# Three stacked half terms per head for the score products of batches 2 to 4

## The reference

```
for t in range(S):
    m_new = maximum(f[t] + m, i[t]); f_stab = exp(f[t] + m - m_new); i_stab = exp(i[t] - m_new)
    C = f_stab * C + i_stab * outer(v[t], k[t]);  n = f_stab * n + i_stab * k[t]
    y[t] = sigmoid(o[t]) * (C @ q[t]) / maximum(abs(n . q[t]), 1)
h = relu(x^T @ w_tok1) @ w_tok2;  u = x + h^T;  out = u + relu(u @ w_ch1) @ w_ch2
```

## Time and profile before

| | |
|---|---|
| median of three runs | 459.25 us (458.14 to 460.07) |
| the profiled execution, its own time | 460.83 us |
| its span, first to last instruction | 459.1 us |
| mean granted TensorE clock | 0.996 |
| PE busy | 440.7 us, 96% |
| DVE / ACT / POOL busy | 259.1 / 209.4 / 209.1 us |
| DMA | 47.38 MB, 103 GB/s on average |
| chain that ended last | PE 83%, issue 6%, DVE 4%, ACT 3%, POOL 2% |

### The profile page before, as it was taken

The page is one execution under the profiler, slowest core; times in us unless marked ns, Lnnn a source line. Parts: engine busy times, 40 slices in busy tenths (PEclk is TensorE's granted clock), DMA queues, the critical chain, the costliest instruction groups (busy, mean ns, idle before and its releaser), DMA issues.

```text
span 459.1 us, 9511 instructions
## 1 busy us (share of the span) xinstructions
PE 440.7 (96%) x3463; PEld 407.9 (89%) x3463; DVE 259.1 (56%) x592; ACT 209.4 (46%) x517; POOL 209.1 (46%) x293
## 2 busy tenths in 40 slices
PE   7899989998999998999999998999999998999996
PEld 3587878998999997999999997899999997999996
DVE  8588965678865346776663236677674326222212
ACT  3665449665555247655552136755552213211120
POOL 7524410888886242988871204698883000000000
PEclk9899999999999999999999999999999999999999
DMA  7666991343344414544344013444410010000101
GB/s 215 191 172 192 348 256 39 104 115 129 95 134 136 140 44 115 148 127 131 127 152 141 1 44 87 144 135 140 126 60 1 1 43 1 0 2 0 45 1 43
DMA packets 36617, 47.38 MB, mean 103 GB/s; under 512 B 3357, under 2 KB 29083, under 8 KB 36571
## 3 DMA queue, kind: packets, MB, share of 16 engines
q1 hardware_dynamic: 35674, 45.76, 33.1%
q10 hardware_dynamic: 896, 1.02, 0.6%
HBM read 42.73 MB, written 4.03 MB: 102 GB/s over the span
## 4 chain that ended last, share of the span: by engine, by line
PE 83%; issue 6%; DVE 4%; ACT 3%; POOL 2%; DMA 1%; ACTq 0%; DVEq 0%; POOLq 0%
PE pC L1151 32%; PE pA L1222 7%; PE pA L1223 7%; PE pA L1224 7%; PE pS L1063 6%; PE pA L1151 5%; PE pY L1120 4%; PE pA L1226 3%; PE pA L1227 3%; PE pY L1099 2%; PE pN L1075 2%; DMA x<-o_gate_dram 1%; PE pA L1181 1%; POOL vw L517 1%; DVE pb L860 1%
## 5 line engine op out<-in xcount | busy, mean ns | idle before, releaser
L974 DVE SCALAR_TENSOR_TENSOR h_lo<-pA,h_hi 128x384 fp32r<-128x384 f32 x96 | 53.5, 557 | 148.0 <-ACT h_hi L755 147.9
L755 ACT ACTIVATE h_hi<-pA 128x384 fp32r<-128x384 f32 x96 | 46.9, 489 | 138.7 <-PE pA L1227 138.6
L1151 PE MATMUL pC<-wc_hi,h_hi 128*128 128x320 f32 x288 | 94.1, 327 | 0.8 <-DVE wc_lo L841 0.8
L1151 PE MATMUL pC<-wc_lo,h_hi 128*128 128x320 f32 x288 | 88.7, 308 | 0.0
L1151 PE MATMUL pC<-wc_hi,h_lo 128*128 128x320 f32 x288 | 88.5, 307 | 0.0
L489 POOL TENSOR_TENSOR gb<-gb,pb 128x384 f32<-128x384 f32 (+1 forms) x54 | 51.7, 957 | 65.7 <-ACT pb L623 65.4
L1222 PE MATMUL pA<-uT_hi,wc_hi 128*128 128x384 f32 x192 | 65.3, 340 | 1.9 <-DVE uT_hi L952 1.9
L1223 PE MATMUL pA<-uT_lo,wc_hi 128*128 128x384 f32 x192 | 64.7, 337 | 0.0
L1224 PE MATMUL pA<-uT_hi,wc_lo 128*128 128x384 f32 x192 | 64.3, 335 | 0.0
L1151 PEld LDWEIGHTS pC<-wc_hi,h_hi 128*128 128x128 f32 x288 | 54.0, 188 | 2.1 <-DVE h_lo L974 1.1
L1151 PEld LDWEIGHTS pC<-wc_lo,h_hi 128*128 128x128 f32 x288 | 54.2, 188 | 0.1
(11 more groups left out here) (128 smaller groups left out, 885.0 us busy)
## 6 DMA issues: line engine op xcount, KB each, us to landing
gb<-g_dram SPq DMA_DIRECT2D x18, 512.0 KB, 4.0
kv<-kvN_dram SPq DMA_DIRECT2D x24, 324.0 KB, 4.1
kd<-kT_dram SPq DMA_DIRECT2D x24, 180.0 KB
qz<-qT_dram SPq DMA_DIRECT2D x72, 60.0 KB
out_dram<-u SPq DMA_DIRECT2D x24, 160.0 KB, 1.9
qd<-qT_dram SPq DMA_DIRECT2D x20, 180.0 KB, 2.6
gq<-g_dram SPq DMA_DIRECT2D x45, 60.0 KB
wc_raw<-w_ch_dram SPq DMA_DIRECT2D x6, 384.0 KB, 5.8
```

The lines of the kernel that those rows point to most:

```text
L755: nc.scalar.activation(h2[0][:, slot % 2], pA[slot % 2][:, 0:HALF], ACT.Relu).then_inc(h2_hi, 1)
L974: nc.vector.scalar_tensor_tensor(h2[1][:, slot % 2], pA[slot % 2][:, 0:HALF], 0.0, h2[0][:, slot % 2].bitcast(F32), ALU.max, ALU.subtract) ...
L1151: ins = mm(dst, a[p], b[q], start=first and n == 0, stop=last and n == 2)
```

## The change

Batch 0 keeps the plain product. For batches 1 to 3 the host lays keys and queries out a second time (array kq): per head 120 rows, which hold the 40 components three times over, the middle copy split around row 64, as `order` says. On the chip the whole 120 rows are rounded to fp32r (kq_stack), then rows 0 to 39 of the keys and rows 64 to 103 of the queries are overwritten with their low halves (raw minus rounded). One fp32r product over 120 rows then sums key-low x query-high, high x high and key-high x query-low. It is one product of 128 x 128 per head, three (or two) per step, in place of one float32 product of 384 (or 256) columns.

```diff
+FIRST_PREPARED = 3
+PREPARES_AT = 2
+TWO_AT = 6
+K_LOW, Q_LOW = slice(0, D), slice(64, 64 + D)
...
-        gq = sb("gq", [ROWS, Q, NG, L])
+        gq = sb("gq", [ROWS, R, NG, L])
+        kq_raw = sb("kq_raw", [ROWS, NG, 2, GH, L])
+        kq_stack = sb("kq_stack", [ROWS, NG, 2, GH, L], F32R)
...
+        def prepares(ba, m):
+            if m < PREPARES_AT:
+                return []
+            steps = [m + 1] if m < TWO_AT else [m + 1, m + 2] if m == TWO_AT else [m + 2]
+            n = STEPS + (FIRST_PREPARED if ba < B - 1 else 0)
+            return [later(ba, k) for k in steps if k < n and later(ba, k) >= FIRST_PREPARED]
...
+            def load_step(ba, m):                      # SP
+                c, g = divmod(m, NG)
+                k = later(ba, m)
+                if k < NG:
+                    sp.wait_ge(s_mm, STEPS)
+                elif k < NG + FIRST_PREPARED:
+                    sp.wait_ge(kq_first, 2 * (k - NG + 1))
+                else:
+                    sp.wait_ge(kq_lo, k - NG - FIRST_PREPARED + 1)
+                    sp.wait_ge(kq_low_keys, k - NG - FIRST_PREPARED + 1)
+                sp.dma_start(kq_raw[:, g], kq[ba - 1, c, :, g]).then_inc(kq_in[g], 16)
...
+            def load_two_steps(ba, c):
+                load_step(ba, NG * c)
+                load_step(ba, NG * c + 1)
             def load_rest(ba, c):
-                if ba > 0:
-                    load_decays(ba, c)
                 load_values(ba, c)
+                load_decays(ba, c)
+                load_step(ba, NG * c + 2)
                 if c > 0:
-                    load_inter(ba, c)
+                    load_query_decays(ba, c)
+                    load_queries(ba, c)
             def load_chunk(ba, c):
-                load_scores(ba, c)
+                load_two_steps(ba, c)
                 load_rest(ba, c)
...
             def rest(ba, m):                           # POOL
+                sixteen_bits(ba, m)                    # the old body of rest
+                for k in prepares(ba, m):
+                    low_keys(k)
+            def low_keys(k):
+                raw, stack = step_tiles(kq_raw, k % NG), step_tiles(kq_stack, k % NG)
+                pool.wait_ge(kq_hi, k - FIRST_PREPARED + 1)
+                nc.gpsimd.tensor_tensor(stack[0][K_LOW], raw[0][K_LOW], stack[0][K_LOW].bitcast(F32),
+                                        ALU.subtract).then_inc(kq_low_keys, 1)
...
+                    if n == NC:                        # ahead of batch 1's first rest
+                        for m in range(FIRST_PREPARED):
+                            prepare_first(m)           # copy 120x768 and both low halves, all on POOL
...
+                for k in prepares(ba, m):              # ACT, in attention(ba, m), after chunk_start and v_middle
+                    step_high(k)
+            def step_high(k):
+                g = k % NG
+                act.wait_ge(kq_in[g], 16 * (k // NG + 1))
+                act.wait_ge(s_mm, STEPS + k - NG + 1)
+                nc.scalar.activation(kq_stack[:, g, :, 0:HEADS[g], :], kq_raw[:, g, :, 0:HEADS[g], :],
+                                     ACT.Copy).then_inc(kq_hi, 1)
...
+                    for k in prepares(ba, m):          # DVE, in attention(ba, m), after p_low(m-1)
+                        step_low(k)
+            def step_low(k):
+                raw, stack = step_tiles(kq_raw, k % NG), step_tiles(kq_stack, k % NG)
+                dve.wait_ge(kq_hi, k - FIRST_PREPARED + 1)
+                nc.vector.tensor_tensor(stack[1][Q_LOW], raw[1][Q_LOW], stack[1][Q_LOW].bitcast(F32),
+                                        ALU.subtract).then_inc(kq_lo, 1)
...
+            def step_scores(ba, m):                    # PE, from batch 1 on
+                g = m % NG
+                k = later(ba, m)
+                if k < FIRST_PREPARED:
+                    pe.wait_ge(kq_first, 2 * (k + 1))
+                else:
+                    pe.wait_ge(kq_lo, k - FIRST_PREPARED + 1)
+                    pe.wait_ge(kq_low_keys, k - FIRST_PREPARED + 1)
+                pe.wait_ge(p_ready, STEPS + k)
+                for j in range(HEADS[g]):
+                    last = mm(scores_bank(ba, m)[:, j * L:(j + 1) * L], kq_stack[:, g, 0, j, :], kq_stack[:, g, 1, j, :],
+                              start=True, stop=True)
+                last.then_inc(s_mm, 1)
...
+        order = np.r_[0:D, 0:64 - D, 0:D, 64 - D:D]    # host
```

More of the change, by code:

```diff
@@ L163, in program, with gq_at, step_tiles @@
         pN = bank("pN")
+        def gq_at(ba, c):
+            if ba == 0:
+                return gq_first[:, :, :] if c % Q == R else gq[:, c % Q]
+            return gq[:, c % R]
+        def step_tiles(tensor, g):
+            return [tensor[:, g, side, 0:HEADS[g], :] for side in range(2)]
         def scores_bank(ba, m):
@@ L179, in program @@
         gb_in = [sem(f"gb_in{i}") for i in range(Q)]
-        gq_in = [sem(f"gq_in{i}") for i in range(Q)]
+        gq_in = [sem(f"gq_in{i}") for i in range(R)]
+        kq_in = [sem(f"kq_in{i}") for i in range(NG)]
+        kq_hi = sem("kq_hi")
+        kq_lo = sem("kq_lo")
+        kq_low_keys = sem("kq_low_keys")
+        kq_first_hi = sem("kq_first_hi")
+        kq_first = sem("kq_first")
         g_out = sem("g_out")
@@ L416, in _ @@
                 if b < B - 2:
-                    load_scores(b + 2, 0)
+                    load_two_steps(b + 2, 0)
                 store(b, 0)
@@ L562, in attention @@
                         x_low(ba, c - 1)
+                for k in prepares(ba, STEPS):
+                    low_keys(k)
                 x_low(ba, NC - 1)
@@ L1125, in attention @@
             def attention(ba, m):
-                if m < STEPS:
+                if m < STEPS and ba > 0:
                     step_scores(ba, m)
                 if ba == 0:
+                    if m < STEPS:
+                        first_scores(m)
                     if m in (1, 4):
@@ L1265, in rows, with stacked @@
         return np.ascontiguousarray(padded.reshape(B, NG, ROWS, NC, L).transpose(0, 3, 2, 1, 4))
+    def stacked(a):
+        order = np.r_[0:D, 0:64 - D, 0:D, 64 - D:D]
+        heads = np.concatenate([a[1:], np.zeros((B - 1, NG * GH - H, S, D), np.float32)], axis=1)
+        return heads.reshape(B - 1, NG, GH, NC, L, D).transpose(0, 3, 5, 1, 2, 4)[:, :, order]
     def by_partition(w, k):
```

127 lines of the change are left out of this document (77 added, 50 removed).

## The result

The changed kernel takes **546.4 us** (median; 543.0 to 546.7) beside 459.7 for the kernel before (458.1 to 460.4): a ratio of 1.188, 95% interval 1.182 to 1.193. The forecast was 466 with a range of 451 to 480. The direction was right, the size was not: +87 us in place of +7. (The title counts the batches from 1: its batches 2 to 4 are batches 1 to 3 of this text.)

What follows compares the result with a forecast made beforehand. PE was taken as the bound, POOL becoming the pace: POOL's ends 5.3, 7.2 and 6.2 us later, less 3.65 each, give 7.75; minus 1.0 is +6.7 on the 459.25 median, so 466 us, range 451 to 480.

Steps and rivals of the forecast that it cites:

- What bounds the kernel before: PE, busy 96% of the span; POOL second, with 11 to 13 us to spare in each batch's long window.
- Part 1: PE's score steps, batches 1 to 3: narrow products at 0.10 us each save 16.7 us of PE work.
- Part 4: Outside the windows: 1.0 us saved in token mixing; prepare_first costs nothing; ACT and DVE keep 14 us or more spare.
- Part 2: POOL's added subtraction per step, 0.98 or 0.70 us, makes POOL the pace, ending at least 1.3, 3.2 and 2.2 us later.
- Part 3: POOL idles 4 us per batch at step 3 onward, gb and gq loads, so ends 5.3, 7.2 and 6.2 us later.
- The cover of 3.65 us: In each batch POOL may end 3.65 us later before PE, at step_values(17), ends later than now.
- A: POOL never idle in the windows: 454 us, chance 0.14; full version, subtraction at 0.35 us or less: 443, chance 0.08.
- B: POOL idle near 1.8 us per batch, so gain and loss cancel: 458 to 461 us, chance 0.15.
- C: PE's narrow product costs 0.215 us, no less than before: 467 us, chance 0.12.
- D: POOL and DVE hinder each other, wide subtractions 1.25 us: 475; or PE's clock falls behind scores(3): 472; chance 0.10.
- E: Load queue sets the pace, gb or gq late by 1.5 us at eight later chunks: 478 us, chance 0.08.
- The signs: If right: PE idle longest at step 3, POOL idle under 8 us per window, PE busy down 14 to 17 us.

Runs made afterwards that it cites:

- c3: c1 with the narrow 128-column products as plain float32 in place of fp32r: 514.1 us.
- c1: Changed kernel with batch 1's output gate load early, step_high directly behind p_high, kv, gb and gq loads ahead of kq, two-step-ahead preparation from step 2: 511.7 us.
- c6: c5, but SP's loads in the changed kernel's order except the gate early and only gq moved ahead of each chunk's third kq load: 506.9 us.
- e1: Changed kernel with the load of batch 1's output gate issued ahead of that batch's second chunk: 529.2 us.
- e4: Changed kernel with ACT's step_high moved directly behind p_high, ahead of the chunk's border work and v_middle: 528.5 us.
- e3: Changed kernel without DVE's subtraction of the queries' low halves and its waits, that term left out: 527.2 us.
- c7: c6 without POOL's subtraction of the keys' low halves, that term left out: 483.4 us.
- c8: c6 without both subtractions, POOL's and DVE's, both low terms left out; copies and loads stay: 468.0 us.
- c16: c6 without DVE's subtraction of the queries' low halves, that term left out: 490.2 us.
- e2: Changed kernel without POOL's subtraction of the keys' low halves and its waits, that term left out: 510.8 us.
- e5: Changed kernel with six dummy bfloat16 products of 512 columns per step on PE, ahead of its wait for the low halves: 547.2 us.
- c17: c6 with two dummy bfloat16 products of 512 columns per step on PE: 507.4 us.
- e7: Changed kernel with each chunk's kv, gb and gq loads issued ahead of its three kq loads: 534.9 us.
- c5: c1 with DVE's values ahead of p_low and step_low: 507.1 us.

## Why the prediction was wrong

By its own parts.

**What bounds the kernel before: right.** PE, at 96%. (By the page's totals DVE comes next; the forecast took POOL, which is fuller in its windows.)

**Part 1, right, and worth nothing.** A narrow product costs 0.097 us where 0.10 was taken. The forecast's sum had already left this gain out, but for Part 4's 1.0 us, as POOL was to be the pace. c3 bears that out for c1, where 12.8 us more on PE cost 2.4.

**Part 2, nearly right in its work, wrong in its bearing.** POOL's work in the three windows is 69.6, 67.4 and 66.2 us, where the forecast has 64.6, 63.6 and 62.7. The subtraction took 1.24 us wide and 0.80 narrow in place of 0.98 and 0.70 (POOL's groups by shape in the changed kernel):

```profile
L596 POOL TENSOR_TENSOR kq_stack<-kq_raw,kq_stack 40x384 fp32r<-40x384 f32 x34 | 42.0, 1236 | 18.5 <-ACT kq_stack L753 18.5
...
L596 POOL TENSOR_TENSOR kq_stack<-kq_raw,kq_stack 40x256 fp32r<-40x256 f32 x17 | 13.6, 803 | 1.0 <-ACT kq_stack L753 1.0
```

34 x 0.26 + 17 x 0.10 are 10.5 us over all batches, no more. But POOL did not become the pace: a chunk lasts 15.4 to 19.4 us in batch 2, where POOL's work was to ask for 13.1 and asks for 13.7.

**Part 3 is the step that failed: "idle time that POOL can't shed", 4 us per batch.** The waits it names are all there and near their prices: PE's wait at scores(3) (3.9 us forecast, 4.22 in batch 2), POOL's for gb at chunks 2 and 3 (1.6 and 0.5 forecast, 1.50 and 0.74 in batch 2), and low_keys(6), held up behind gq (1.1 forecast, 2.38). What it put at almost nothing is the rest: POOL "loses little, some 0.2 each" on the way round, and the later chunks lose nothing. In batch 2 POOL's rests waited 8.3 us for p_high, and its subtraction about 1 us for step_high once in each later chunk. So POOL was idle 16.0, 17.1 and 17.4 us where 4 was written, and its end came 22.3, 24.1 and 23.2 us later where the forecast has 5.3, 7.2 and 6.2. The cover of 3.65 us took little off that: PE was itself held up all the way, and step_values(17) of batch 2 came 3.61 us behind the last cast in place of 4.26, so 0.65 was absorbed.

Each wait was priced by itself, on a clock taken from the kernel before, as if the others ran on time. In the queues' order ACT's copy, the two halves, PE, SP's loads and ACT's copy again close a ring, in which what one loses the next starts from; that this ring made the small waits large is my reading, as no run opened it at one place alone. What runs show is that order matters: the order edits (c6), with every instruction kept, take 39.5 of the 87 us back. They include e1's, worth 17.2 alone, which belongs to Part 4.

**Part 4 failed twice.** "prepare_first ... costs nothing" looked at what stands behind it on POOL (rest(0), for which POOL was free in time, at 76.7) and not at who waits for it: SP, and behind SP the gate's load. 17.2 us (e1), more than any other edit of the order but e4's 17.9, and it was nowhere; rest(0) was late after all, by 14.5 us, through the gate. And "ACT gets 51 copies, DVE 51 subtractions ... which leaves 14 and more": spare time is no cover in a queue that works in order. DVE's subtractions are 34.8 us of work and 54.2 us of standing in front of them; the place of ACT's copy alone was worth 17.9 (e4), and taking the subtractions out 19.2 (e3). DVE's added work itself costs 15.4 to 16.7 once the order is mended (c7 to c8, c6 to c16), although DVE has 2.5 us to spare in a chunk of 15.3.

**The rivals.** A (POOL keeps up) and B have nothing for them. C fell with Part 1's number. D's price for POOL came true (1.24 us for a wide subtraction, 1.02 in e3 without DVE's), and is some 9 us of POOL's work. On the other side, DVE's wide p_low takes 0.97 us on the mean, 0.85 before and 0.79 in e2, but not by meeting POOL's subtraction: none of the 36 ran beside one. Six took 2.02 us or more, and all six began while POOL was at scale_q (L604) or the low piece of the values (L656), with the next rest right behind, as the one at 268.31 did. Where p_low began 0.03 us ahead of rest, it was POOL that lost, 1.30 us in place of 0.92 (both timelines):

```profile
233.27 0.55 DVE L974 TENSOR_TENSOR pb<-gb,pb 128x384 bf16<-128x384 f32 x1
```

```profile
233.30 1.30 POOL L565 TENSOR_TENSOR gb<-gb,pb 128x384 f32<-128x384 f32 x1 [1.79 <-ACT pb L727]
```

The Trainium skill (SBUF — State Buffer, "SBUF: two separate sides") says that whichever of the two starts first keeps the port pair for the whole instruction and the other is blocked; these rows agree on who loses. The 0.38 us that rest lost here are less than p_low's 0.55; the p_low at 268.31 lost 1.47 us beside 1.64 us of L656 and L565. The fall of the clock that D priced came, in more places than it named, and e5 and c17 show no time given back when PE is kept at work and the mean clock is higher; neither separates the clock from the work that raises it. E (loads behind low halves at every chunk) was nearest, at 478, with 0.08. That e7 gave 11.5 us against its 12 is chance: POOL waited for gb five times in all (12.6 us, 8.1 of them ahead of batch 1's attention), otherwise only at chunks 2 and 3, as the forecast had it.

**The signs.** Right were PE's longest wait at scores(3) of batches 2 and 3 (4.22 and 4.21 us, though the profile names no releaser there), chunks of 12.9 us and more, and POOL's waits for gb. Wrong were POOL's idle time (16 to 17 us, "under 8") and PE's busy time, which rose by 17.6 us at the lower clock in place of falling by 14 to 17.

**The account**, from 546.4 to 460.3: order of queues and loads 39.5 (546.4 to c6), POOL's subtraction 23.5, DVE's 15.4, and 7.7 for what then remains: copies, kq's loads and c5's order, less what PE gains. The parts depend on the order in which they are taken away (POOL's subtraction is 35.6 from the changed kernel, 23.5 from c6, 2.9 from c1). How the last 7.7 divides between the ACT copies, the 13 MB more of loads and DVE's order was not tried. No version here beats the kernel before; the best that computes everything is c6, a single run at 1.10 of its time.

## What to carry to other kernels

When a change adds a wait to an engine that works in order, list everything queued behind it and go on from each item to its own waiters until the list closes; if it comes back to the start, price the ring, not the links. That an engine has spare time says nothing about it: DVE was 54% busy, and its added subtractions still cost 19 us. And look at a load queue for what has nothing to do with the change: one of the two costliest places here was that of an output gate.

## What the runs showed of the hardware that was not expected

- A three-head step of fp32r products of 128 columns over 120 rows takes 0.29 us, 0.097 a product, and the same products as plain float32 (c3) 0.66 us (241.14 to the next product at 241.80), about the 0.65 of the one wide float32 product before. So three narrow float32 products cost what one wide one did, and the gain comes from the format:

```profile
241.14 0.83 PE L1212 MATMUL pS<-kq_stack 120*128 120x128 f32 x6
241.80 0.38 PE L1224 MATMUL pN<-vw,kv 128*120 128x123 f32 x2
```

- DVE's wide p_low ran from 0.54 to 2.42 us with the same shape in one execution of the changed kernel, by what POOL was doing when it began; a single row of it is no price.
- 47 us more of PE's busy time went into the waits of the changed kernel for less than 1 us of time, with the mean granted clock at 0.978 in place of 0.927 (e5).
